# A four-batch attention and two-layer MLP kernel: shorter GpSimd instructions, one-port small operations, longer load rows in batch 0, and a new order

## The reference

```python
# attention: pooled (every 4 tokens averaged, 144 of them) plus banded (|i-j| < 4)
out_d = sm_attn(mean4(q), mean4(k), mean4(v)); out_up = np.repeat(out_d, 4, axis=2)
scores = np.where(abs(i - j) < 4, scale * q @ k.T, -1e9)
x = out_up + softmax(scores) @ v                  # -> (4, 576, 512)
# mixing by Fourier transform over tokens and features, layer norm, MLP 512 -> 2048 -> 512
u = x + real(fft(fft(x, axis=1), axis=2))
x = u + relu(((u - mean(u)) / sqrt(var(u) + 1e-6)) @ w_ch1) @ w_ch2
# gated MLP 512 -> 1024 -> 512 with a convolution of three taps over tokens
h = relu(x @ w_in); out = (h * sigmoid(conv3(h, conv_w))) @ w_out
```

## Time and profile before

| | |
|---|---|
| median of three runs | 878.08 us |
| time of the profiled execution | 877.0 us |
| its span, first to last instruction | 875.1 us |
| TensorE busy | 845.3 us (97%) |
| VectorE, ScalarE, GpSimd busy | 454.6, 309.0, 251.1 us |

### The profile page before, as it was taken

How to read it: one execution, slowest core, us unless ns; L and a number is a source line. 1 busy time by engine, 2 the same in 40 slices (tenths; PEclk the granted TensorE clock), 3 DMA queues, 4 the chain that set the end, 5 groups by cost and what they waited for, 6 DMA issues and landing times.

```text
span 875.1 us, 17508 instructions
## 1 busy us (share of the span) xinstructions
PE 845.3 (97%) x7162; PEld 787.1 (90%) x7162; DVE 454.6 (52%) x870; ACT 309.0 (35%) x942; POOL 251.1 (29%) x288
## 2 busy tenths in 40 slices
PE   8797999999999999999979999999999999999998
PEld 7675789999999898899979999999999889898996
DVE  4668964566543635675541222222245857567563
ACT  4545354255423442332231212122232444334332
POOL 3657973355611742400000242424242000000000
PEclk9988989999999999999998999999999999999999
DMA  9932331314310303110005000011010010010101
GB/s 231 242 89 57 72 74 38 94 44 108 74 49 2 82 1 121 50 72 25 25 27 221 31 31 31 31 31 31 31 31 1 1 49 1 1 62 1 49 1 60
DMA packets 76617, 49.75 MB, mean 57 GB/s; under 512 B 60289, under 2 KB 65689, under 8 KB 76538
## 3 DMA queue, kind: packets, MB, share of 16 engines
q1 hardware_dynamic: 74826, 44.37, 19.0%
q10 hardware_dynamic: 1712, 4.26, 1.3%
HBM read 39.18 MB, written 9.45 MB: 56 GB/s over the span
## 4 chain that ended last, share of the span: by engine, by line
PE 86%; DVE 6%; SPq 2%; ACT 1%; DMA 1%; issue 1%; POOL 1%; DVEq 0%; ACTq 0%
PE banks L770 23%; PE banks L787 23%; PE banks L890 12%; PE banks L873 10%; PE banks L731 2%; PE banks L678 2%; PE banks L704 2%; PE banks L607 2%; PE banks L593 2%; PE banks L746 2%; PE banks L640 2%; PE banks L626 1%; PE banks L663 1%; PE banks L652 1%; PE banks L757 1%
## 5 line engine op out<-in xcount | busy, mean ns | idle before, releaser
L1238 DVE SCALAR_TENSOR_TENSOR hL<-banks,hH 128x256 fp32r<-128x256 f32 x144 | 60.8, 422 | 201.8 <-ACT hH L989 201.6
L989 ACT ACTIVATE hH<-banks 128x256 fp32r<-128x256 f32 x144 | 55.3, 384 | 263.9 <-PE banks L770 263.7
L1531 POOL TENSOR_TENSOR astage<-astage,rstd_bc 128x1024 f32<-128x1024 f32 x9 | 21.6, 2400 | 241.1 <-DVE astage L1367 241.1
L770 PE MATMUL banks<-unH,w1aH 128*128 128x256 f32 x288 | 86.2, 299 | 0.1
L787 PE MATMUL banks<-hH,w2aH 128*128 128x256 f32 x288 | 84.0, 292 | 0.0
L770 PE MATMUL banks<-unH,w1bH 128*128 128x256 f32 x288 | 82.4, 286 | 0.0
L770 PE MATMUL banks<-unL,w1aH 128*128 128x256 f32 x288 | 82.1, 285 | 0.0
L770 PE MATMUL banks<-unH,w1aL 128*128 128x256 f32 x288 | 82.1, 285 | 0.0
L770 PE MATMUL banks<-unH,w1bL 128*128 128x256 f32 x288 | 82.0, 285 | 0.0
L770 PE MATMUL banks<-unL,w1bH 128*128 128x256 f32 x288 | 82.0, 285 | 0.0
L787 PE MATMUL banks<-hH,w2bH 128*128 128x256 f32 x288 | 81.9, 284 | 0.0
(11 more groups left out here) (174 smaller groups left out, 2275.6 us busy)
## 6 DMA issues: line engine op xcount, KB each, us to landing
qk_in<-in_q SPq DMA_DIRECT2D x32, 144.0 KB, 2.6
qk_in<-in_k SPq DMA_DIRECT2D x32, 144.0 KB, 3.2
v_grp<-in_v SPq DMA_DIRECT2D x16, 288.0 KB
acc_dram<-astage SPq DMA_DIRECT2D x9, 512.0 KB, 3.3
astage<-acc_dram SPq DMA_DIRECT2D x9, 512.0 KB, 3.3
out<-ostage SPq DMA_DIRECT2D x16, 256.0 KB, 2.3
v_win<-in_v SPq DMA_DIRECT2D x32, 122.5 KB
w2araw<-in_moe_w_ch SPq DMA_DIRECT2D x4, 512.0 KB, 6.3
```

The lines of the kernel that those rows point to most:

```text
L770: last = nc.tensor.matmul(bank[0][:, 0:CT], w[wp][:, t, P * m:P * m + P], (unH, unL)[xp][:, t, :], start=(t == 0 and i == 0), stop=(t == P ...
L989: nc.scalar.activation(hH[:, m % 2, :], bank[0][:, 0:CT], ACT.Relu).then_inc(hH_ok, 1)
L1238: nc.vector.scalar_tensor_tensor(hL[:, m % 2, :], bank[0][:, 0:CT], 0.0, hH[:, m % 2, :].bitcast(F32), ALU.max, ALU.subtract).then_inc(hL_ ...
L1531: nc.gpsimd.tensor_tensor(astage[:], astage[:], rstd_bc[:].unsqueeze(1).to_broadcast([P, PB, CT]), ALU.mult).then_inc(scaled, 1)
```

## The change

The edits, with the diff cut to its core below:

- Batch 0 only: q and k are loaded in rows of 1,536 B per head (six tokens in one partition), one DMA for both heads. The transposes then take strided token tiles: per tile one transpose for the first head and one ordinary matmul with the identity for the second, and the copies out of PSUM put the tokens back in order.
- All pairs: one copy out of PSUM for q and one for k, in place of two each; `flip_q` and `flip_k` are no longer split into halves.
- `pool_q` of batch 0 moves from three GpSimd additions to one VectorE reduction.
- The two small VectorE operations per pair: 1e-9 is no longer added by a scalar addition over `sums`. `sums` has a second column set to 1e-9 once, and a reduction over two columns makes the sum. `top_d` writes its maxima into PSUM, and the negation reads them from there.
- GpSimd: `fold_d` in two halves (288 columns in place of 576, four instructions in place of two), `low_w1` in four instructions of 256 columns in place of one of 1,024.
- ScalarE runs one exponential on constants at the very start.
- `PLAN` is another order of the same steps. 42 `warm` matmuls in place of 60. Of the eight weight loads all but the last two now stand ahead of `load_q.2`. `low_w1.0.0` to `low_w1.0.2` stand between pairs 2 and 4 and `low_w1.0.3` inside `feat.0`; before, all four stood behind `fold.3` or later. Both `wmeans.0` stand ahead of `flip_q.4` (before: one). `vars.1` and `vars.2` stand further behind `square.1` and `square.2`; the last batch's statistics stand as before.

```diff
@@ start of PLAN @@
-    load_q.0 load_k.0 load_c.0 load_w2.0.0 load_vg.0 warm.15 flip_q.0.0 load_w1.0.0 flip_q.0.1 keep_q.0.0 load_q.1
-    keep_q.0.1 pool_q.0 warm.2 flip_k.0.0 flip_k.0.1 keep_k.0.0 load_k.1 keep_k.0.1 pool_k.0 warm.2 score.0.0
+    load_q.0 load_k.0 load_vg.0 load_vw.0 warm.6 flip_q.0 load_vw.1 keep_q.0 warm.2 flip_k.0 pool_q.0 load_q.1
+    pool_v.0 load_c.0 keep_k.0 load_k.1 load_c.1 pool_k.0 warm.2 score.0.0 load_vg.1 score_d.0 load_w1.0.0 score.0.1
+    load_c.2 top_d.0 exp_d.0 load_w2.0.0 load_w1.0.1 load_w1.0.2 warm.7 flip_q.1 load_w1.0.3 load_w2.0.1 mask.0.0
+    keep_q.1 load_q.2 top_l.0.0 mask.0.1 load_w2.0.2 exp_l.0.0 warm.2 flip_k.1 top_l.0.1 load_w2.0.3 pool_q.1 load_k.2
@@ between the last join of batch 0 and feat.0 @@
-    flip_p.4.0 join.3.1 load_vw.5 round_w1.0.2 score.5.0 norm_d.4 fold.3 flip_p.4.1 round_w1.0.3 low_w1.0.0 score.5.1
-    keep_p1.4 fold_d.0.1 round_w2.0.3 low_w1.0.1 mask.5.0 warm.7 feat.0.0.0 mask.5.1 top_l.5.0 feat.0.0.1 keep_cos.0.0
+    exp_l.4.1 weigh.3.0 keep_k.5 load_k.6 join.3.0 score.5.0 pool_k.5 weigh.3.1 round_w1.0.3 score.5.1 join.3.1
+    load_vw.5 pool_q.5 fold.3 norm_l.4.0 warm.5 score_d.5 invert.4.1 fold_d.0.1 norm_l.4.1 flip_p.4.0 norm_d.4
+    flip_p.4.1 keep_p1.4 keep_p0.4 feat.0.0.0 top_d.5 pool_v.4 feat.0.0.1 keep_cos.0.0 exp_d.5 mask.5.0 feat.0.1.0
...
+    q_row = q.rearrange("b (c two) (p t) d -> (b c) p two (t d)", two=2, t=NT)
...
             def load_q(n):
-                at_least(sp, q_flipped, 2 * n)
+                at_least(sp, q_flipped, n)
+                if n < PB:
+                    sp.dma_start(qk_row[:, 0], q_row[n]).then_inc(q_loaded, 16)
+                    return
...
+            def flip_tiles(n, which):
+                for t in range(NT):
+                    g, j = divmod(t, HT)
+                    cols = slice(QT * j, QT * j + QT)
+                    if n >= PB:
+                        tile = qk_in[:, which, t].rearrange("p two d -> p (two d)")
+                        last = nc.tensor.transpose(T[:, g, cols], tile, ident[0:QT, 0:QT])
+                        continue
+                    tiles = [qk_row[:, which, h, Dh * t:Dh * t + Dh] for h in range(2)]
+                    nc.tensor.transpose(T[0:Dh, g, cols], tiles[0], ident[0:QT, 0:QT])
+                    last = nc.tensor.matmul(T[Dh:P, g, cols], tiles[1], ident[0:QT, 0:QT], start=True, stop=True)
...
+                nc.scalar.mul(token_tiles(n, 0), flipped_tiles(n), SCALE).then_inc(q_kept, 1)
...
+                nc.vector.tensor_copy(token_tiles(n, 1), flipped_tiles(n)).then_inc(k_kept, 1)
...
+            def pool_q(n):    # VectorE, pairs 0 to 3
+                dve.wait_ge(q_kept, n + 1)
+                at_least(dve, d_scored, n)
+                nc.vector.tensor_reduce(q_pool[:, 0:Sd], qkT[:, 0, :].rearrange("p (i r) -> p i r", r=FACTOR),
+                                        AX.X, ALU.add).then_inc(q_pooled, 1)
...
-                nc.vector.tensor_scalar(sums_e[n % 2][:, cols], sums[n % 2][:, cols], 1.0e-9, None, ALU.add).then_inc(sum_eps, 1)
+                nc.vector.tensor_reduce(sums_e[n % 2][:, cols], sums[n % 2][:, cols], AX.X, ALU.add).then_inc(sum_eps, 1)
...
+                halves = (slice(0, HS), slice(HS, S))
+                for cols in halves:
+                    nc.gpsimd.tensor_tensor(plus[:, 0, cols], xs[:, 0, cols], xs[:, 2, cols], ALU.add).then_inc(g_p, 1)
...
+                for t in range(PB):    # low_w1
+                    nc.gpsimd.tensor_tensor(low[:, t], raw[:, t], high[:, t].bitcast(F32), ALU.subtract).then_inc(w1L_ok[half], 1)
...
+            act.wait_ge(consts_set, 1)
+            nc.scalar.activation(ntop_d[0][:, 0:1], mean_of[:, 0:1], ACT.Exp)
```

More of the change, by code:

```diff
@@ L84 @@
[L84 to L98, removed]
@@ L109 @@
[L109 to L118, removed]
@@ new lines @@
+    mask.1.1 warm.2 flip_pd.0 exp_l.1.0 top_l.1.1 keep_cw warm.1 wmeans.0.0 exp_l.1.1 invert.1.0 norm_l.1.0 keep_pd.0
+    invert.1.1 norm_d.1 round_w2.0.0 flip_q.2 centre_w1.0.0 norm_l.1.1 pooled.0 low_w2.0.0 keep_q.2 load_q.3 keep_up.0
+    flip_k.2 round_w2.0.1 pool_q.2 weigh.0.0 round_w1.0.0 keep_k.2 load_k.3 pool_k.2 score.2.0 low_w1.0.0 mask.2.0
+    score_d.2 top_l.2.0 join.0.0 flip_p.1.0 exp_l.2.0 flip_p.1.1 keep_p0.1 weigh.0.1 pool_v.2 top_d.2 score.2.1
+    keep_p1.1 load_vw.2 exp_d.2 mask.2.1 flip_pd.1 join.0.1 top_l.2.1 fold.0 keep_pd.1 load_vg.3 invert.2.0 low_w2.0.1
@@ new lines @@
+    exp_l.2.1 warm.3 flip_q.3 centre_w1.0.1 pooled.1 load_q.4 keep_up.1 norm_l.2.0 keep_q.3 invert.2.1 warm.1
+    weigh.1.0 norm_l.2.1 round_w1.0.1 flip_k.3 pool_q.3 norm_d.2 join.1.0 round_w2.0.2 weigh.1.1 keep_k.3 load_k.4
+    low_w1.0.1 round_w2.0.3 pool_k.3 score.3.0 load_vw.3 score.3.1 mask.3.0 top_l.3.0 score_d.3 mask.3.1 exp_l.3.0
+    pool_v.3 flip_p.2.0 top_d.3 flip_p.2.1 top_l.3.1 wmeans.0.1 exp_d.3 keep_p0.2 invert.3.0 load_vg.4 keep_p1.2
+    join.1.1 norm_l.3.0 exp_l.3.1 low_w2.0.2 fold.1 flip_pd.2 low_w2.0.3 keep_pd.2 warm.3 flip_q.4 pooled.2 invert.3.1
@@ new lines @@
+    keep_q.4 load_q.5 centre_w1.0.2 keep_up.2 flip_k.4 norm_l.3.1 weigh.2.0 load_k.5 keep_k.4 round_w1.0.2 norm_d.3
+    join.2.0 warm.1 flip_p.3.0 pool_q.4 flip_p.3.1 keep_p0.3 weigh.2.1 pool_k.4 score.4.0 keep_p1.3 load_vw.4 join.2.1
+    low_w1.0.2 flip_pd.3 mask.4.0 top_l.4.0 score_d.4 centre_w1.0.3 keep_pd.3 exp_l.4.0 flip_q.5 fold.2 top_d.4
+    score.4.1 load_q.6 mask.4.1 exp_d.4 top_l.4.1 invert.4.0 keep_q.5 warm.4 pooled.3 flip_k.5 keep_up.3 fold_d.0.0
+    exp_l.4.1 weigh.3.0 keep_k.5 load_k.6 join.3.0 score.5.0 pool_k.5 weigh.3.1 round_w1.0.3 score.5.1 join.3.1
@@ new lines @@
+    contract.1.6 split.1.7 keep_q.11 load_q.12 norm_l.10.1 round_u.2.1 round_u.2.2 low_u.2.1 pool_q.11 flip_k.11
+    round_u.2.3 pooled.9 keep_k.11 load_k.12 keep_up.9 pool_k.11 flip_p.10.0 pool_v.11 weigh.9.0 low_u.2.2 flip_p.10.1
+    score.11.0 keep_p0.10 score.11.1 join.9.0 low_u.2.3 load_vg.12 weigh.9.1 mask.11.0 expand.2.0 join.9.1 keep_p1.10
+    load_vw.11 top_l.11.0 fold.9 mask.11.1 exp_l.11.0 flip_pd.10 top_l.11.1 score_d.11 keep_pd.10 invert.11.0 top_d.11
+    relu.2.0 flip_q.12 norm_l.11.0 contract.1.7 split.2.0 keep_q.12 load_q.13 exp_d.11 pool_q.12 flip_k.12 keep_acc.1
@@ new lines @@
+    keep_q.13 load_q.14 norm_l.12.1 norm_d.12 flip_k.13 pool_q.13 expand.2.4 keep_k.13 load_k.14 pool_k.13 flip_p.12.0
+    relu.2.4 flip_p.12.1 split.2.4 pooled.11 contract.2.3 keep_up.11 pool_v.13 expand.2.5 load_vg.14 weigh.11.0
+    relu.2.5 contract.2.4 keep_p0.12 join.11.0 split.2.5 weigh.11.1 expand.2.6 join.11.1 keep_p1.12 load_vw.13 fold.11
+    flip_pd.12 relu.2.6 contract.2.5 keep_pd.12 fold_d.2.1 flip_q.14 split.2.6 feat.2.0.0 load_q.15 feat.2.0.1
+    keep_cos.2.0 feat.2.1.0 keep_sin.2.0 feat.2.1.1 keep_cos.2.1 feat.2.2.0 keep_sin.2.1 feat.2.2.1 keep_cos.2.2
```

302 lines of the change are left out of this document (151 added, 151 removed).

## The result

The changed kernel takes 891.65 us (median of four runs, 890.18 to 892.70); the kernel before, run beside it, takes 878.84 us (four runs, 876.96 to 883.91). The ratio is 1.0135, 95% interval 1.0089 to 1.0182: slower by 1.35%, and outside the predicted range. The profiled execution took 892.7 us, with a span of 890.5.

What follows compares the result with a forecast made beforehand. TensorE was taken as the bound (86% of the chain), with gains mostly before 120 us. Gains of 24.1 minus 7.2 and 3.2 left 13.7 us off 877.0; with the median 1.1 higher, 864.5 us, 8 in 10 within 853 to 877.

Steps and rivals of the forecast that it cites:

- What it costs: Batch 0's eight flips: 0.6 us for added matmuls and 0.3 us later copies, 7.2 us lost; one slow-clock spell, 3.2 us.
- The copy: Copies out of PSUM in batch 0: one instead of two starts later, some 0.3 us per flip.
- The start, 3.8 us: Before the first transposes: early table load gains 1.28 us, longer rows land q 2.5 us earlier.
- The loads, 8.9 us: Load of k of pair 3: long rows remove waits of 0.84 and 3.46 us and 4.6 us of slow clock.
- the second rival: Loads stay the bound: DMA full by bytes and order, not pieces; the 8.9 us don't come, 873.5 us; chance 0.14.
- The last fold, 5.9 us: Wait before feat.0: 4.3 of 6.3 us gained as GpSimd stops blocking VectorE, plus 1.6 us of slow spell.
- 96 to 120, 3.1 us: TensorE waits of 1.3 and 1.8 us from 96 to 120 us go; the 3.2 us slow spell stays.
- Statistics: The vars waits: two go (1.2 us) with slow pieces behind (1.3 us), 2.4 us gained; the last, 3.7 us, stays.
- a sign of being wrong: Idle time of TensorE between 120 and 400 us, listed among the observations that would show the forecast wrong.
- The clock: First 120 us: slow spells of 4.6 and 1.6 us won back, one of 3.2 us charged for fewer warm matmuls.
- The rival of that name: Fewer warm matmuls, then long waits, keep the clock low over the first 70 us: 27 us more, 891; chance 0.08.

Runs made afterwards that it cites:

- run 2: The changed kernel with q and k of batch 0 in the old short rows, six-transpose flips and contiguous copies; 870.58 us, ratio 0.9915.
- run 3: The changed kernel with head 0 of batch 0 also flipped by matmul, the two heads by turns, no transposes; 871.55 us, ratio 0.9911.
- run 6: The changed kernel with all-matmul flips in batch 0, all six tiles of head 0 before those of head 1; 873.78 us, ratio 0.9926.
- runs 8 and 9: The changed kernel alternating full-width matmuls with transposes (874.68 us), then full-width with half-width matmuls and no transposes (907.39 us).
- run 12: The changed kernel with short rows and transpose flips, plus q and k loads of pair 2 ahead of the last weight loads; 863.92 us, ratio 0.9812.
- run 13: The changed kernel, flips still alternating, with q and k loads of pair 2 moved ahead of later weight loads; 890.79 us, ratio 1.0104.
- runs 11, 12: The changed kernel with pair 2's q and k loads ahead of the last weight loads: with all-matmul flips 864.48 us, with short rows 863.92 us.
- run 15: The changed kernel with all-matmul flips and early pair 2 loads, its small VectorE operations and short GpSimd instructions undone; 866.31 us, ratio 0.9838.
- run 10: The changed kernel with more warm matmuls, fifteen for six before the first flip and eleven for seven before pair 1's; 889.19 us, ratio 1.0098.
- run 8: The changed kernel with head 1's matmuls at full width, the transpose of head 0 writing over the lower half; 874.68 us, ratio 0.9957.

## Why the prediction was wrong

**The step that failed** is the first of "What it costs": "Each flip of batch 0 gets twelve more short matmul instructions of 96 columns ... 0.44 to 0.93 us, I take 0.6". A flip of six transposes takes 0.7 us; the changed one takes 3.1, or 4.9 at the low pace. With the copy the term was 7.2 us. The flips cost 32.6 us where eight short ones cost 7.6 (run 2), so 25 in place of 4.8. Two things were missing. I priced the new instructions by groups in which all are alike and never the change from one to the next: eleven changes of 0.13 us are 1.46 us a flip at the full pace. And those groups write for the two heads by turns, to both halves of the partitions, where runs 3 and 6 show instructions side by side. The new ones all go to one half: twelve at 0.083 us are 1.0 us and not 0.6. The two together are 2.46 us, and 3.12 - 0.66 is what the flip gained. The Trainium skill, "TensorEngine Tiling (Array Packing)" (Key Properties), says that changing the tiling mode drains TensorE, and (Restrictions) that column tiling excludes the transpose mode for float32. Together they name what costs here; the runs 8 and 9 bear them out, with 0.13 to 0.16 us a change at the full pace. This was the rule that spoke against the change, and I did not weigh it.

**The copy** was to be 0.3 us later. The reordering copies of batch 0 take 1.19 us each on either engine. In the kernel before, a copy by a free engine ended about 0.5 us (q of pair 2) to 0.6 us (k of pairs 0 to 2) behind its flip; in the changed kernel it ends 1.2 us behind. That is 0.6 to 0.8 us later, about 5 to 6 us over the eight, where the term had 2.4. Against the unordered copies of run 2 (0.65 and 0.76 us) it is 3.9 us.

A check that uses only measured terms: from run 2 to the changed kernel the flips add 25.0 us and the copies 3.9, and the waits for q and k fall from 6.4 to 0.8 us. That is 23.3 us; measured are 21.1.

**The start, 3.8 us.** The signs came: the table load at 1.17 us, the first transpose at 4.83 in place of 7.11. But the 2.5 us for q had the wrong cause. The landings of the first load of q, short rows before and long rows after, and the first flip of run 2, which has short rows:

```profile
DMA to landing us min/median/max: 3.2/3.3/3.5
...
DMA to landing us min/median/max: 4.0/4.0/4.0
...
4.45 1.19 PE L607 MATMUL banks<-ident,qk_in 96*128 96x96 f32 x6 [0.46 <-DMA qk_in<-in_q]
```

The short rows were issued at 0.74 and 1.19 us and had landed at 4.67; the long row, issued at 0.74, landed at 4.69. Before, TensorE did not wait for q at 7.11 us: it was still busy with its thirty `warm` instructions. Twelve of them in place of thirty brought the 2.3 us, not the longer rows. The first scores nevertheless began at 17.45 us in place of 10.98. With short rows and early loads (run 12) they began at 8.05: 2.9 us of the 3.8 are there when the flips are cheap.

**The loads, 8.9 us.** No wait for k was left, but because TensorE came late (run 13). The term went to the wrong cause. In the changed kernel the load of k of pair 2 landed at 41.8 us and its flip began at 47.97. With short rows in the new order 6.4 us of waits for q and k stay (run 2); moving two loads wins 7 us with either kind of row (runs 11, 12). What was full was the queue by its order: the second rival's mechanism, which I gave 0.14. Long rows do relieve the engines somewhat: from 20 to 40 us their share is 0.85 with them (run 3) and 0.99 without (run 2), at 252 and 258 GB/s. With the cheap flips of run 3 this about pays for the flips and copies (871.55 against 870.58 us).

**The last fold, 5.9 us, and 96 to 120, 3.1 us.** The wait before `feat.0` fell to 0.2 us, below the 2 us that I left. Run 15 says that the order did it. The small operations are as said (158 and 161 ns on average) and, together with the short GpSimd instructions, worth 1.8 us in run 15, no more than its uncertainty.

**Statistics.** Right: only the last `vars` waits, 3.7 us. Not foreseen were small waits for `sum` (0.7 us) and hL (1.6 us in all). They are part of the idle time between 120 and 400 us, which the prediction had named as a sign of being wrong; run 2 has 1.9 us of the same two.

**The clock.** Busy time times (1 - clock) is 12.3 us over the first 120 us against 10.2 before: 2 us lost. I had counted on 4.6 and 1.6 us back and charged 3.2, a gain of 3.0. The rival of that name gave 891, the number that came, by a mechanism that run 10 refutes; the agreement is chance.

**The rest of the change** gains. Without long rows (run 2) it gives 7.5 us by the ratio, where my sum without the loads' term and the flips' (24.1 - 8.9 - 3.2) has 12.0. What each part of the order brings was not tested.

## What to carry to other kernels

Price a new instruction in the place where it will stand: a group of equal ones says nothing of what a change between neighbours costs. In float32, transposes and full matmuls are one width of the array, matmuls to 64 partitions another; keep each width together, or send both heads through the narrow form by turns, where the halves work side by side. Before making transfers faster, try moving the few that are waited for ahead of those that are not: here that gave 7 us in the new order and 3.5 in the old. And look whether the engine that seems to wait for a load is not still busy with filler work of its own.

## What the runs showed of the hardware

- A change of array width costs 0.13 us between a float32 transpose and narrow matmuls, whether they change by one tile or by two (1, 5, 9 and 11 changes in a flip: 1.79, 2.32, 2.86, 3.12 us), 0.17 us at the low pace, and 0.16 us between wide and narrow matmuls. A change between transpose and matmul at the same width costs nothing that shows (run 8).
- Float32 matmul instructions of 96 columns start every 0.083 us on one half of the output partitions. With the two halves by turns, one starts every 0.041 us: a flip of 24 takes 1.22 us (run 3) against 1.89 (run 6).
- At the start TensorE works at the low pace while its granted clock is written as 1.00: in the changed kernel four `warm` instructions take 1.22 us at 9.66 and 1.23 us at 16.01, and four take 0.71 us at 26.34. In run 12 the first flip, at 4.50 us, was already at the full pace (0.69 us), with the same `warm.6` ahead of it as in run 2, where the first flip took 1.19 us. What decides between them stays open.
